# First tile of a blocked linear-attention scan: inverse from 16x16 blocks, solved per chunk, and later weight loads

## The reference

```python
k_n = k / (np.linalg.norm(k, axis=-1, keepdims=True) + 1e-06)
for t in range(S):
    kt, vt, bt = (k_n[:, :, t], v[:, :, t], beta[:, :, t, None])
    y[:, :, t] = np.einsum('bhd,bhde->bhe', q[:, :, t], state)
    v_old = np.einsum('bhde,bhd->bhe', state, kt)
    state = state + bt[:, :, :, None] * np.einsum('bhd,bhe->bhde', kt, vt - v_old)
x = y.transpose(0, 2, 1, 3).reshape(3072, 384)
h = np.maximum(x @ w_in, 0.0);  x = h * h @ w_out                 # 384 -> 2048 -> 384
h = np.maximum(np.maximum(x @ w1, x @ w2), x @ w3); out = h @ w_out2   # 384 -> 768 -> 384
```

## Time and profile before

| | |
|---|---|
| median of 3 runs | 949.91 us |
| the profiled execution | 946.07 us |
| its span, first to last instruction | 944.1 us |
| TensorE busy | 868.9 us (92%) |
| VectorE busy | 428.9 us (45%) |
| GpSimd busy | 285.4 us (30%) |
| ScalarE busy | 265.8 us (28%) |
| mean granted TensorE clock | 0.969 |

### The profile page before, as it was taken

The page is one execution under the profiler, slowest core; times in us unless marked ns, Lnnn a source line. Parts: engine busy times, 40 slices in busy tenths (PEclk is TensorE's granted clock), DMA queues, the critical chain, the costliest instruction groups (busy, mean ns, idle before and its releaser), DMA issues.

```text
span 944.1 us, 20905 instructions
## 1 busy us (share of the span) xinstructions
PE 868.9 (92%) x9148; PEld 743.6 (79%) x9148; DVE 428.9 (45%) x641; ACT 265.8 (28%) x464; POOL 285.4 (30%) x392
## 2 busy tenths in 40 slices
PE   2326699999999999999999999999999999999998
PEld 2326588878888888888888888887898989898988
DVE  6936365574566456645544444434323232323231
ACT  2211343233223322332233233633222222122221
POOL 4147898813941394139400000721000000000000
PEclk8658899999999999999999999999999999999999
DMA  7976764165424532353223134012020202010000
GB/s 185 220 142 148 160 148 102 52 138 132 106 60 97 131 105 60 93 129 80 64 63 91 36 95 123 9 51 67 1 67 1 67 1 67 0 67 1 34 1 34
DMA packets 123435, 76.27 MB, mean 81 GB/s; under 512 B 94320, under 2 KB 107120, under 8 KB 123344
## 3 DMA queue, kind: packets, MB, share of 16 engines
q1 hardware_dynamic: 121088, 73.89, 31.7%
q10 hardware_dynamic: 2256, 1.05, 0.4%
HBM read 53.18 MB, written 20.45 MB: 78 GB/s over the span
## 4 chain that ended last, share of the span: by engine, by line
PE 89%; DMA 3%; DVE 3%; SPq 3%; issue 1%; ACT 0%; ACTq 0%; DVEq 0%
PE psum L71 25%; PE psum L73 24%; PE psum L72 24%; PE psum L667 3%; PE psum L605 2%; PE psum L591 2%; PE psum L616 2%; PE psum L655 2%; PE psum L674 2%; PE psum L631 1%; PE psum L642 1%; DMA dram_f<-sol_f 1%; SPq L372 1%; DMA kz_first<-in_kT 1%; SPq L326 1%
## 5 line engine op out<-in xcount | busy, mean ns | idle before, releaser
L967 DVE TENSOR_TENSOR sq<-relu 128x512 f32<-128x512 f32 x96 | 76.2, 793 | 151.2 <-ACT relu L1103 151.1
L73 PE MATMUL psum<-x_lo,wb 128*128 128x512 f32 x324 | 126.3, 390 | 0.0
L72 PE MATMUL psum<-x_hi,wb 128*128 128x512 f32 x324 | 126.3, 390 | 0.0
L71 PE MATMUL psum<-x_hi,wb 128*128 128x512 f32 x324 | 126.2, 389 | 0.0
L71 PE MATMUL psum<-x_hi,win 128*128 128x512 f32 x288 | 116.3, 404 | 9.0 <-DVE x_lo L956 7.9
L1103 ACT ACTIVATE relu<-psum 128x512 f32<-128x512 f32 x96 | 57.3, 597 | 228.6 <-PE psum L73 228.6
L104 POOL TENSOR_TENSOR sol_tmp<-sol_b,sol_f 128x31 f32<-128x31 f32 (+15 forms) x155 | 90.1, 581 | 84.6 <-DMA sol_b<-dram_b 72.7
L71 PE MATMUL psum<-sq_hi,wout 128*128 128x512 f32 x288 | 114.2, 396 | 1.0 <-DVE sq_lo L972 1.0
L72 PE MATMUL psum<-x_hi,win 128*128 128x512 f32 x288 | 113.2, 393 | 0.0
L73 PE MATMUL psum<-x_lo,win 128*128 128x512 f32 x288 | 113.1, 393 | 0.0
L73 PE MATMUL psum<-sq_lo,wout 128*128 128x512 f32 x288 | 112.4, 390 | 0.0
(11 more groups left out here) (99 smaller groups left out, 1280.0 us busy)
## 6 DMA issues: line engine op xcount, KB each, us to landing
kz<-in_kT SPq DMA_DIRECT2D x40, 192.0 KB, 3.5
v_t<-in_vn SPq DMA_DIRECT2D x12, 384.0 KB, 3.5
qa<-in_qT SPq DMA_DIRECT2D x24, 192.0 KB, 3.8
nz<-in_kn SPq DMA_DIRECT2D x24, 192.0 KB, 4.3
x2T<-x SPq DMA_DIRECT2D x6, 768.0 KB, 4.1
x_raw<-x2T SPq DMA_DIRECT2D x6, 768.0 KB, 4.6
out_dram<-o_t SPq DMA_DIRECT2D x24, 192.0 KB, 1.9
raw_wb<-in_w SPq DMA_DIRECT2D x18, 192.0 KB, 4.4
```

Of the source, the lines that this page charges most:

```text
L71: nc.tensor.matmul(out, lhs_hi, rhs_hi, start=first, stop=False)
L72: nc.tensor.matmul(out, lhs_lo, rhs_hi, start=False, stop=False)
L73: return nc.tensor.matmul(out, lhs_hi, rhs_lo, start=False, stop=last)
L967: nc.vector.tensor_tensor(d.sq[:], d.relu[:], d.relu[:], ALU.mult).then_inc(s.sq_ready, 1)
```

## The change

For tile 0 alone the 32x32 blocks are replaced by 16x16 blocks. Each chunk has 4 x 2 x 16 = 128 of these, one a partition, so each chunk is solved by itself (substitute_small, chunk 0 and then chunk 1, both on VectorE). Two products (x_small, g_small) join 16x16 blocks to 32x32 ones, in both forms that later products use (f_nat, n_nat), and two more (x_first, g_first) join those to 64x64. Both parts of kk, take_kk, sums and norms of tile 0 run per chunk. Keys of the first four chunks are stored without zeros beside them (k_nat), and the products of tile 0 use only the 48, 64 or 32 partitions that hold data. Stores and loads of the small blocks are shared between SP's and ScalarE's queues. The rows of tiles 1 and 2 now use one buffer, and the rows of tile 2 are loaded after load_blocks(1). Of the weights only pieces 0 and 1 are loaded in the head; 2 to 7 are loaded after place_last_heads(0). split_low of piece 0 stays on GpSimd, those of 1 to 7 go to VectorE inside the dense loop of tile 0; split_high of 2 to 7 stands in f = 1 to 6 there. FIRST_PLAN is changed. The core of the diff (SP has store_small and spread_small for h = 0, like ScalarE's for h = 1; x_first and g_first are x_block and g_block on 32 partitions):

```diff
-FIRST_PLAN = Plan(1, 10, 13, 15, 18, 21, 23, 26, 27, 28, 29)
+FIRST_PLAN = Plan(1, 13, 15, 17, 19, 21, 23, 25, 26, 27, 29)
...
+def substitute_small(eng, ops, link_sem, at, b, f, tmp, one, solved):
...
+    updated = [at, at]
+    for r in range(QUART - 1, 0, -1):
+        cut = (r + QUART + 1) // 2
+        parts = [(r, cut), (cut, QUART)] if cut < QUART else [(r, QUART)]
+        taken = []
+        for i, (c0, c1) in enumerate(parts):
+            eng.wait_ge(link_sem, updated[i] if len(parts) > 1 else updated[-1])
+            part = tmp[:, i, 0:r * (c1 - c0)].rearrange("p (j i) -> p j i", j=r)
+            shape = [P, r, c1 - c0]
+            taken.append(linked(ops.tensor_tensor(part, b[:, 0:r, r:r + 1].broadcast_to(shape),
+                                                  f[:, r:r + 1, c0:c1].broadcast_to(shape), ALU.mult)))
+        updated = []
+        for i, (c0, c1) in enumerate(parts):
+            eng.wait_ge(link_sem, taken[i])
+            part = tmp[:, i, 0:r * (c1 - c0)].rearrange("p (j i) -> p j i", j=r)
+            updated.append(linked(ops.tensor_tensor(f[:, 0:r, c0:c1], f[:, 0:r, c0:c1], part, ALU.subtract)))
+        updated += updated[-1:] * (2 - len(parts))
+    eng.wait_ge(link_sem, updated[-1])
+    ops.tensor_tensor(b.rearrange("p i j -> p j i"), f, one.broadcast_to([P, QUART, QUART]), ALU.mult).then_inc(solved, 1)
+    return count[0]
...
-    START_HI = 3
+    START_HI = 2
+    POOL_LOW = 1
...
-            sp.dma_start(d.beta_all[:].rearrange("p (n u) -> p n u", n=CYCLES), beta.rearrange("n p u -> p n u")).then_inc(s.beta_in, 16)
-            sp.wait_ge(s.kz_zero, 1)
-            load_k(0, False)
+            load_k_first(0)
+            sp.dma_start(beta_of(0), beta[0]).then_inc(s.beta_in, 16)
             load_k_first(1)
+            sp.dma_start(beta_of(1, CYCLES), beta[1:].rearrange("n p u -> p n u")).then_inc(s.beta_more, 16)
             load_v(0)
+            sp.wait_ge(s.cg_ready, 1)
+            store_small(0, 0)
+            load_small(0)
+            sp.wait_ge(s.cg_ready, 2)
+            store_small(1, 0)
             sp.wait_ge(s.qa_zero, 1)
             load_q(0)
-            sp.wait_ge(s.cg_ready, 1)
-            store_blocks(0, BLOCKS, s.b0_stored)
-            sp.wait_ge(s.cg_ready, 2)
-            store_blocks(1, BLOCKS[:2], s.b0_stored)
-            load_blocks(0)
+            load_small(1)
+            sp.wait_ge(s.q1_zero, 1)
+            load_q(1)
+            sp.dma_start(rows[:], kn[1]).then_inc(s.rows_in, 16)
+            sp.wait_ge(s.solved_small, 1)
+            sp.dma_start(small_f[0].rearrange("b s p j i -> (b s p) j i"), sol_of[0][1]).then_inc(small_f_stored[0], 16)
+            sp.wait_ge(s.nat_zero, 4)
+            spread_small(0, 0)
             load_swapped(0)
-            sp.dma_start(rows_of[1][:], kn[1]).then_inc(s.rows_in1, 16)
             load_k_first(2)
+            sp.wait_ge(s.solved_small, 2)
+            sp.dma_start(small_f[1].rearrange("b s p j i -> (b s p) j i"), sol_of[1][1]).then_inc(small_f_stored[1], 16)
+            spread_small(1, 0)
             load_k_first(3)
-            store_beside(0, s.o0_stored)
-            store_beside(1, s.o0_stored)
+            load_v(1)
             sp.wait_ge(s.nz_zero, 1)
             load_kn(0)
             load_piece(0)
             load_piece(1)
-            load_piece(2)
-            sp.wait_ge(s.qk_done, 1)
-            load_k(1, True)
-            load_v(1)
-            sp.dma_start(rows_of[2][:], kn[2]).then_inc(s.rows_in2, 16)
-            sp.wait_ge(s.ob_zero, 3)
-            load_ob(0)
-            sp.wait_ge(s.kk_done, 4)
-            load_piece(4)
-            sp.wait_ge(s.fz_zero, 1)
-            store_f(0)
-            load_f1(0)
-            load_fz(0, [1])
             for c in (2, 3):
                 sp.wait_ge(s.cg_ready, c + 1)
                 store_blocks(c, BLOCKS, s.b_stored)
                 store_beside(c, s.o_stored)
             load_blocks(1)
-            sp.wait_ge(s.x_done, 1)
-            load_ob(1)
-            load_f1(1)
-            sp.wait_ge(s.fd_done, 1)
-            load_fz(1)
-            load_q(1)
+            load_swapped(1)
             load_kn(1)
-            load_swapped(1)
+            sp.wait_ge(s.kz_zero, 1)
+            load_k(4, False)
+            sp.wait_ge(s.ssq_ready, 3)
+            sp.dma_start(rows[:], kn[2]).then_inc(s.rows_in, 16)
+            place_last_heads(0)
+            load_piece(2)
+            load_v(2)
             sp.wait_ge(s.b_stored, B_TILE)
             sp.wait_ge(s.o_stored, O_TILE)
+            sp.wait_ge(s.x_done, 2)
             load_piece(3)
-            sp.wait_ge(s.qk_done, 2)
-            load_k(4, False)
-            load_v(2)
-            place_last_heads(0)
             load_q(2)
             load_kn(2)
             load_swapped(2)
-            for i in range(5, FIRST_WB):
+            for i in range(4, FIRST_WB):
                 load_piece(i)
...
             pool.wait_ge(s.units_ready, 2)
-            pool.wait_ge(s.solved, 1)
-            for i in range(3):
+            pool.wait_ge(s.solved_small, 2)
+            for i in range(POOL_LOW):
                 split_low(i)
-            solve(1)
-            for i in range(3, FIRST_WB):
-                split_low(i)
-            for g in range(2, CYCLES):
+            for g in range(1, CYCLES):
                 solve(g)
...
+            def x_small(c, b):
+                pe.wait_ge(n_nat_in[c], 6 * 16)
+                pe.wait_ge(s.a_ready, 2 * (c + 1))
+                for p in range(PAIRS):
+                    for h in range(2):
+                        for q in range(2):
+                            last = nc.tensor.matmul(bank[third(h, q), b, p * QUART:(p + 1) * QUART],
+                                                    cg_of[c][third(h, q), p, HALF * q:HALF * q + HALF], n_nat[c][third(h, q), p, 0:QUART],
+                                                    start=True, stop=True)
+                last.then_inc(s.x1_done, 1)
+            def g_small(c, b):
+                pe.wait_ge(s.x1_ready, c + 1)
+                pe.wait_ge(f_nat_in[c], 8 * 16)
+                for p in range(PAIRS):
+                    for h in range(2):
+                        for q in range(2):
+                            last = nc.tensor.matmul(bank[third(h, q, QUART), b, p * QUART:(p + 1) * QUART], x_nat[c][third(h, q), p, :],
+                                                    f_nat[c][third(h, q), p, HALF * q + QUART:HALF * q + HALF], start=True, stop=True)
+                for p in range(PAIRS):
+                    for h in range(2):
+                        at = 256 + p * QUART
+                        last = nc.tensor.matmul(bank[third(h, 0), b - 1, at:at + QUART], f_nat[c][third(h, 0), p, 0:HALF],
+                                                x_nat[c][third(h, 0), p, :], start=True, stop=True)
+                last.then_inc(s.g1_done, 1)
...
-            for c in range(4):
-                kk(c, 2 * c)
-            qk(0, 0)
-            x_block(0, 4)
-            g_block(0, 5)
-            f_d(0)
-            x_block(1, 2)
+            for c in range(2):
+                kk_first(c, 2 * c)
+            for c in range(2):
+                qk_first(c, 4 + 2 * c)
+            x_small(0, 4)
+            g_small(0, 5)
+            x_small(1, 6)
+            x_first(0, 4)
+            g_small(1, 7)
+            g_first(0, 5)
+            x_first(1, 6)
+            f_d_first(0, 4)
+            kk_first(2, 0)
             pe.wait_ge(s.sw_zero, 1)
-            y(0)
-            su(0)
-            k_s(1)
-            g_block(1, 3)
-            qk(1, 0)
-            f_d(1)
-            y(1)
-            su(1)
+            y(0, 4)
+            g_first(1, 7)
+            pe.wait_ge(s.g_ready, 4)
+            su(0, 6)
+            kk_first(3, 2)
+            pe.wait_ge(s.y_ready, 2)
+            k_s_first(1, 4)
+            f_d_first(1, 6)
+            y(1, 4)
+            su(1, 6)
+            pe.wait_ge(s.cg_ready, 4)
...
-            unit_matrix(dve, nc.vector, s.dve_link, 0, d.sol_f, zero, one)
-            sums(0)
+            for c in range(2):
+                identity_small(c, 2 * c)
+            dve.wait_ge(s.dve_link, 4)
+            sums_first(0)
             dve.wait_ge(s.beta_in, 16)
-            norms(0)
+            norms(unit_cols(0), 1)
             take_kk(0, 0)
+            sums_first(1)
+            norms(unit_cols(1), 2)
             take_kk(1, 2)
             scale_v(0)
-            dve.wait_ge(s.solb_in, 16)
-            substitute(dve, nc.vector, s.dve_link, 2, d.sol_b, d.sol_f, (d.relu[:, 0:256], d.sq[:, 0:256]), one, s.solved)
+            links_small = 4
+            for c in range(2):
+                dve.wait_ge(small_in[c], 16)
+                links_small = substitute_small(dve, nc.vector, s.dve_link, links_small, *sol_of[c], tmp, one, s.solved_small)
+            dve.wait_ge(s.solved_small, 2)
+            for c in range(2):
```

(98 more changed lines are left out.)

350 lines of the change are left out of this document (238 added, 112 removed).

## The result

The changed kernel takes 965.47 us (median of four runs, 962.89 to 967.41) beside 950.15 for the kernel before on the same chip (947.35 to 952.12): ratio 1.0172, 95% interval 1.0144 to 1.0199. Forecast were 946.0 and a range of 937 to 953.5. It is 15 us slower, not 4 faster, and outside the range.

A forecast was written before the change was run, and what follows sets the result against it. A 104 us head before a dense TensorE, with GpSimd's solve of tile 1 expected to become the bound. Terms: -3.6 at x_block(2), +0.7 for x_block(3)'s f1, -1.0 at tile 0's end = -3.9 us: 946.0, range 937 to 953.5.

The forecast's parts named there:

- Two ways to gain: TensorE after the head: the dense part starts sooner, and nothing in it waits more than before.
- two clocks: Besides TensorE's head, GpSimd's solve of tile 1 sets x_block(2)'s start, with 4.2 us of slack; expected to become the bound.
- The small solves: VectorE, tile 0: two solves of 7.4 us each, done at 31.6 instead of 43.58, a gain of 12 us.
- Spreading: Small-block stores and loads on SP and ScalarE: stores land in 2.5 us, ScalarE free for x_small(0) at about 38.9.
- Joining: TensorE's products from 38.9 us: 23 us at the higher clock, 26 at the lower; cg of chunk 3 at 67.
- From cg of chunk 3 to the first weight product: End of the head: from 67 us through load_blocks(1), rows of tile 2 and y(1) to 95 instead of 104.3.
- The bubble on VectorE: VectorE idle in front of sums(2): some 12 us, the cost of loading tile 2's rows later.
- The solve of tile 1: GpSimd: starts at 75.4, slowed 7 us by 20 more VectorE instructions at 0.35 each, ends at 126.8, 7.9 later.
- Rival 2: Port held whole: 20 instructions at 0.69 are 14 us, solve of tile 1 ends at 134; 953.5 us, chance 0.13.
- x_block(2): TensorE in tile 0: reached at 129.7 to 131, waits 2 to 5 us for f1, allowed at 134.4.
- The lag of the dense part: Splits moved to VectorE put it about 4 us behind over n=2 to 5; about 2 us reach TensorE.
- Rivals: TensorE stays the bound (941, 0.25); port held whole (953.5, 0.13); nothing to measure or rows load late (949 each, together 0.27).

The follow-up runs named there:

- e2: Changed kernel, only the rows of tile 2 loaded before the stores of chunks 2 and 3, not behind load_blocks(1): 962.23 us, ratio 1.0140.
- e4: Changed kernel with the FIRST_PLAN of the kernel before, x_block(2) at half iteration 10 instead of 13: 971.73 us, ratio 1.0225.
- b1: Kernel before, weight pieces 2 and 4 loaded behind the head, splits two pieces ahead instead of three: 944.19 us, ratio 0.9933.
- b3: b1 with the norms of tile 1 moved into VectorE's wait for the first solve's blocks: 938.06 us, ratio 0.9883 to the kernel before.
- e1: Changed kernel, loads of k of chunk 3, v, kn and weight pieces 0 and 1 held until g_first(0) is done: 966.61 us, ratio 1.0167.
- e5: Changed kernel, only weight pieces 0 and 1 held until g_first(0) is done: 960.50 us, ratio 1.0109.
- after: The changed kernel itself, against the kernel before: 965.47 us, ratio 1.0172.
- b2: Kernel before with low parts of weight pieces 3 to 7 moved from GpSimd to VectorE: 949.49 us, ratio 0.9998.
- e7: e6 with low parts of weight pieces 1 to 7 back on GpSimd behind its solve: 954.72 us, ratio 1.0045.
- e6: Changed kernel, tile 1's norms, kk and cg ahead of the join, tile 2's rows and held pieces behind load_blocks(1), piece 0 split on VectorE: 954.56 us, ratio 1.0050.

## Why the prediction was wrong

**The bound.** Two ways to gain, two clocks: that held. e2 moved the one and met the other, e4 the second alone. The head in front of the join I read half rightly. I wrote that the solved blocks come back late behind the weight pieces, and b1 bears that out: without two of the pieces their store is issued 2.9 us sooner and lands in about 5 us instead of 9.8. What I missed is what hangs on that store. The row at 62.64 names cg_first, not a DMA: TensorE waited there for the norms of tile 1, these for ScalarE's root, and the root stood behind the loads of fz that wait for the store. b1 made the store sooner and gained 6 us, b3 took the norms off this chain and gained 11, both at the old solve. The solve ended at 43.58, but SP came to the store only at 47.16; that a sooner inverse alone would have gained anything was not tried.

**The small solves.** Their length was right: the copies are 7.15 us apart (26.03, 33.18), 7.4 forecast. They end at 33.77 and not at 31.6, since the first starts at 19.34 where the sum had 16.6.

**Spreading.** ScalarE takes x_small(0) at 43.17, not 38.9: +4.3, of which 2.2 come from the solves' late end. The store of f takes 3.4 to 4.0 us to land where I took 2.5, twice in series.

**Joining: the step that failed.** From ScalarE free to cg of chunk 3 I counted 28 us, and it was 41.6 (43.17 to 84.77). Up to 11.3 of the 13.5 us more are TensorE's stops at issue, of which the sum had none: it had no term for the supply of instructions. The kernel before gave no such row to price it by. The one stop at issue in its head, 2.1 us at L616, is another kind: it ends at 84.08, 0.10 us behind VectorE's sw, and so is a plain wait. I wrote that weights no longer stand ahead of the join, and did not price them beside it: e1 took 6.1 us off the two long stops by holding the loads, e5 4.4 us off one of them by holding the two pieces alone, with 5 us in the medians. That the loads cause the long ones is shown by these two runs. That the stops are late instructions is shown by their places: in after and e1 to e5 they stand at the same four products of the sequence, 127 to 128 apart, and in all eight kernels with this join each of the four ends 1.3 to 1.7 us behind a packet of the instruction queue. Those of 1 to 2 us stay with the loads held, because a packet then comes every 3.4 to 4.0 us and its 128 products take 1.9 to 2.8. Why the packets are not sent sooner no run shows. The clock was at its lower level from 40 to 72 us, which I had as the upper bound.

**From cg of chunk 3 to the first weight product.** 28 us forecast, 32.75 measured (84.77 to 117.52): the rows of tile 2 took 7.2 us from issue to use, not 5.0, and y(1) 3.68 us at the lower clock, not 2.1. The bubble on VectorE, 12 us forecast, was 13.62. So the head's miss is 4.3+13.5+4.7 = 22.5 us: 95 for 117.5.

**The solve of tile 1.** I let the moved splits lengthen it by 7 us. It took 42.8 us with its 5 low parts (42.3 before), because the dense part had started late too. The price of one, 0.35 us, was about right: at most 0.31 in e2. The count of 20 was not. Rival 2, by which the port is held for each whole instruction, was wrong as a sum. The pair of rows in b1 shows such a hold once: 1.80 us for 0.18. By the Trainium skill ("SBUF — State Buffer", "SBUF: two separate sides"), quoted in the prediction, the one of VectorE and GpSimd that starts second waits for the whole instruction of the other, if VectorE's has two SBUF inputs or runs in its two-port mode. The rows agree for that pair, though they don't tell the mode of this instruction. e2's 0.31 us at most for each says that GpSimd does not pay the full length every time; VectorE pays as well, with 3.3 and 3.7 us for the two groups beside the solve in after, where the later groups take 1.9.

**x_block(2).** Forecast was a wait of 2 to 5 us; in after there is none. It is reached at 153.42, with f1 issued at 149.47: both clocks were late by nearly the same. The wait stands one step on, at x_block(3): 2.22 us, where the sum had 0.7 for f1 queued on SP, and the clock falls behind it. The slack that the later plan gave is real, 6 us by e4.

**The lag of the dense part.** 2 us forecast for the splits. In after TensorE waits 1.2 us more for relu and 1.5 for a low part of win, 2.7 together, beside two groups of splits that take 3.3 and 3.7 us during the solve: about right. b2, with five groups on VectorE, and e7 against e6 show no difference in time, and in neither do the groups meet the solve of tile 1. No run has after's late solve with the low parts elsewhere, so that their meeting is the cause is argued, not shown. The rest of the 8.5 us is the 2.5 us more at x_block and the 3.8 us of slower products, which the sum did not have.

**Rivals.** None of the four held. All of them put the first weight product at 95 to 103. The one that was missing is "the join takes longer than the solve saves": 640 more products (9788 for 9148), each at the lower clock, with TensorE's stops between them.

## What to carry over

Before making a step on the critical path shorter, follow the row of the engine that waits behind it to the one that it names, and from there on until a DMA or a queue is reached. Here it led from cg_first over the norms of the next tile and ScalarE's root to a store behind a weight piece; moving the norms into a gap that was there, with two weight pieces later, gave 1.2% where a new algorithm lost 1.7%. Many tiny products are no cheap way to shorten a serial step: price them at the lower clock and by the supply of instructions, here one packet for 128 products every 3.4 to 4.0 us, and far later if bulk loads run at the same time. If two chains set two marks, ask for each edit what it does to both: e2's first weight product came 12.8 us sooner, and of that 8.7 us were left in the profiled span and 3 in the median, which is within noise. A stop put down to issue has to be looked into: here it was late instructions, a load that had just landed, or another engine's result.
